# Three chunks of 512 tokens in place of four of 384, units of four query tiles, and the second batch's keys and values loaded late

## The reference

```python
k_sum = k.reshape(B, H, nb, block, D).max(axis=3)
v_sum = v.reshape(B, H, nb, block, D).mean(axis=3)
scores_l = scale * np.matmul(q, k.transpose(0, 1, 3, 2))        # only |i - j| < 16
scores_s = scale * np.einsum('bhsd,bhnd->bhsn', q, k_sum) + np.log(block)
a = softmax(concat(scores_l, scores_s)); x = a @ concat(v, v_sum)

h = np.maximum(x @ w_in, 0.0);  x = h * h @ w_out               # width 2048 inside
h = x @ w_in                                                     # second MLP, width 1024
solu = h * softmax(h)
ln = (solu - mean(solu)) / np.sqrt(var(solu) + 1e-06) * g_ln
out = ln @ w_out
```

## Time and profile before

| | |
|---|---|
| median of three runs | 483.61 us |
| profiled execution | 483.07 us |
| its span, first to last instruction | 481.3 us |
| TensorE busy | 474.0 us, 98% |
| VectorE / ScalarE / GpSimd busy | 253.7 / 207.4 / 30.9 us |
| bytes by DMA | 39.73 MB |
| first up(2) (end of the head) | 33.6 us |
| last `down` ahead of the second MLP ends | 331.6 us |

### The profile page before, as it was taken

How to read it: one execution, slowest core, us unless ns; L and a number is a source line. 1 busy time by engine, 2 the same in 40 slices (tenths; PEclk the granted TensorE clock), 3 DMA queues, 4 the chain that set the end, 5 groups by cost and what they waited for, 6 DMA issues and landing times.

```text
span 481.3 us, 7844 instructions
## 1 busy us (share of the span) xinstructions
PE 474.0 (98%) x2990; PEld 436.1 (91%) x2990; DVE 253.7 (53%) x517; ACT 207.4 (43%) x525; POOL 30.9 (6%) x60
## 2 busy tenths in 40 slices
PE   7999999999999999999999999999999999999997
PEld 5799999899999999999999999999888888888885
DVE  5888787985443444634443424456574444444450
ACT  3986666544343343533433423334353333333341
POOL 2321000240000000000000000000000000000000
PEclk9999999999999999999999999999999999999999
DMA  8999532223211110411000412121122000000001
GB/s 304 290 351 354 153 97 80 87 73 127 70 31 31 57 30 29 161 33 55 1 1 1 133 44 89 44 89 44 56 76 67 24 31 30 26 23 22 23 22 45
DMA packets 27494, 39.73 MB, mean 83 GB/s; under 512 B 2592, under 2 KB 16832, under 8 KB 27456
## 3 DMA queue, kind: packets, MB, share of 16 engines
q1 hardware_dynamic: 27456, 39.22, 25.2%
HBM read 32.77 MB, written 6.29 MB: 81 GB/s over the span
## 4 chain that ended last, share of the span: by engine, by line
PE 86%; issue 7%; DVE 2%; DMA 2%; SPq 1%; ACT 1%; POOL 0%; POOLq 0%; ACTq 0%; DVEq 0%
PE bank L903 25%; PE bank L931 25%; PE bank L1053 13%; PE bank L1026 12%; PE bank L825 4%; PE bank L880 3%; PE bank L1041 2%; PE bank L850 2%; DMA win_raw<-w_in_t 2%; PE bank L859 1%; DVE solu L783 1%; DVE stat L775 1%; DVE lnT_lo L796 0%; SPq L250 0%; PE bank L831 0%
## 5 line engine op out<-in xcount | busy, mean ns | idle before, releaser
L903 PE MATMUL bank<-x_hi,win_hi 128*128 128x384 f32 x256 | 87.7, 343 | 0.0
L931 PE MATMUL bank<-h_hi,wout_hi 128*128 128x384 f32 x256 | 85.9, 335 | 0.0
L903 PE MATMUL bank<-x_hi,win_lo 128*128 128x384 f32 x256 | 85.7, 335 | 0.0
L931 PE MATMUL bank<-h_hi,wout_lo 128*128 128x384 f32 x256 | 85.6, 334 | 0.0
L903 PE MATMUL bank<-x_lo,win_hi 128*128 128x384 f32 x256 | 85.6, 334 | 0.0
L931 PE MATMUL bank<-h_lo,wout_hi 128*128 128x384 f32 x256 | 85.5, 334 | 0.0
L650 DVE TENSOR_TENSOR sqr<-relu 128x384 f32<-128x384 f32 x64 | 35.7, 558 | 88.2 <-ACT relu L490 87.9
L490 ACT ACTIVATE relu<-bank 128x384 f32<-128x384 f32 x64 | 31.5, 492 | 108.5 <-PE bank L903 108.3
L903 PEld LDWEIGHTS bank<-x_hi,win_hi 128*128 128x128 f32 x256 | 48.1, 188 | 0.5 <-DMA q_sb<-qT 0.3
L903 PEld LDWEIGHTS bank<-x_lo,win_hi 128*128 128x128 f32 x256 | 48.1, 188 | 0.0
L931 PEld LDWEIGHTS bank<-h_lo,wout_hi 128*128 128x128 f32 x256 | 48.1, 188 | 0.0
(11 more groups left out here) (78 smaller groups left out, 705.2 us busy)
## 6 DMA issues: line engine op xcount, KB each, us to landing
q_sb<-qT SPq DMA_DIRECT2D x24, 192.0 KB, 2.8
win_raw<-w_in_t SPq DMA_DIRECT2D x8, 512.0 KB, 11.8
wout_raw<-w_out_t SPq DMA_DIRECT2D x8, 512.0 KB, 12.7
win_raw<-w_t SPq DMA_DIRECT2D x8, 512.0 KB, 3.3
v_ext<-vwin SPq DMA_DIRECT2D x24, 144.0 KB, 2.9
k_raw<-kT SPq DMA_DIRECT2D x8, 400.0 KB, 4.2
out<-o_sb SPq DMA_DIRECT2D x12, 256.0 KB, 2.0
v_first<-vrows SPq DMA_DIRECT2D x4, 384.0 KB, 8.3
```

The costliest lines, as they stand in the source:

```text
L903: last = nc.tensor.matmul(up_bank(n), win[a][:, f * WC + k * P:f * WC + (k + 1) * P], x[b][:, c % 2, k * CH:(k + 1) * CH], start=(k == 0 a ...
L931: last = nc.tensor.matmul(down_bank(d), wout[a][:, f * WC + d * P:f * WC + (d + 1) * P], h[b][:, n % 3, :], start=(f == 0 and a == 0 and b ...
```

## The change

CH becomes 512 and TPU 4, so there are 3 chunks, 48 steps and 24 units, still eight to a chunk. VP becomes 4: the second batch's values come in four parts of twice the size. To make room, the first batch's `k_raw` and `v_first` move under `win_hi`; the second batch's keys (`k_next`, for the summaries only), `v_next` and `v_sum` move under `wout_hi` from tile 7 on; `probs` has two buffers, `q_sb` two, `e_sb` one; `lnT_lo` moves. The windows of the second batch's keys are no longer copied by GpSimd but loaded from memory into `k_ext` (`load_kw`). In PSUM all of `up` from step 2 on uses bank 7, and later units' xT has bank 6 for itself. The copies of weights wait for those who used the space before. The orders written out by hand are redone on all engines, and most weight loads move into SyncE's loop over units. The diff, cut to its core (the buffers' declarations and renamed indices are left out):

```diff
-CH = 384
+CH = 512
...
-TPU = 3
+TPU = 4
...
-VP = 8
+VP = 4
...
-V_AT = {4: 0, 6: 1, 7: 2, 8: 3, 9: 4, 10: 5, 11: 6, 12: 7}
-
-VN_BEHIND = {UPC + 2: (1,), UPC + 3: (2, 3), UPC + 4: (4, 5), UPC + 5: (6,), UPC + 6: (7,)}
+K_AT = {1: 0, 3: 1, 5: 2, 6: 3}
+V_AT = {2: 0, 3: 1, 4: 2, 5: 3}
+KTILES = 7
...
         def up_bank(n):
-            return bank[:, 6 + n % 2, 0:CH]
+            return bank[:, 6 if n == 1 else 7, 0:CH]
...
             def load_q(u):
-                sp.dma_start(q_sb[:, u % PPB, :], qT[u, :, :]).then_inc(q_in[u % PPB], 16)
+                if u >= UPC + 2:
+                    sp.wait_ge(scores_ok, u - 1)
+                sp.dma_start(q_sb[:, u % 2, :], qT[u, :, :]).then_inc(q_in[u % 2], 16)
+
+            def load_kn(p):
+                sp.dma_start(k_next[:, p, :], kT[PPB + p, :, MARGIN:MARGIN + S]).then_inc(kn_in[p], 16)
+
+            def load_kw(u):
+
+                row, p = u // PPB, u % PPB
+                sp.wait_ge(scores_ok, u - PPB + 1)
+                dst = k_ext[:, p, :].rearrange("p (t c) -> p t c", t=TPU)[:, :, NB:KX]
+                at = (row % RB) * UQ
+                flat = kT[PPB + p, :, at:at + UQ].rearrange("p (t c) -> p t c", t=TPU)
+                rows, tiles, _ = [list(x) for x in flat.ap]
+                src = bass.AP(flat.tensor, flat.offset, [rows, tiles, [1, WIN]])
+                sp.dma_start(dst, src).then_inc(kw_in[p], 16)
...
+            load_q(UPC + 2)
+            load_kw(UPB)
+            load_vn(0)
+            sp.wait_ge(attn_ps, UPC)
+            sp.wait_ge(vkept_ok, 1)
+            load_kn(0)
+            load_kn(1)
+            load_q(UPC + 3)
+            load_kw(UPB + 1)
+            load_w(win_raw, w_in_t, 3, win_in)
+            load_w(wout_raw, w_out_t, 2, wout_in)
+            load_kn(2)
+            load_kn(3)
             for u in range(UPC, UNITS):
                 if u >= 2 * UPC and u % UPC == 0:
                     save_y(u // UPC - 2)
                 sp.wait_ge(attn_ps, u + 1)
                 if u + PPB < UNITS:
+                    load_vw(u + PPB)
                     load_q(u + PPB)
-                    load_vw(u + PPB)
-                if UPB - PPB - 3 <= u < UPB - 3:
-                    p = u - (UPB - PPB - 3)
-                    sp.wait_ge(kwin_ok, UPB - PPB + p + 1)
-                    load_k(1, p)
-                for j in VN_BEHIND.get(u, ()):
-                    load_vn(j)
+                if UPB <= u + PPB + 2 < UNITS:
+                    load_kw(u + PPB + 2)
+                if u == UPC:
+                    sp.dma_start(g_sb[:, :], g_cols).then_inc(g_in, 16)
+                    load_vn(1)
+                for g in range(4 + 2 * (u - UPC), min(6 + 2 * (u - UPC), F1 // WG)):
+                    load_w(win_raw, w_in_t, g, win_in)
+                    load_w(wout_raw, w_out_t, g - 1, wout_in)
+                if u == UPC + 1:
+                    load_vn(2)
+                    load_w(wout_raw, w_out_t, F1 // WG - 1, wout_in)
+                if u == UPC + 2:
+                    load_vn(3)
                 if u == UPB - 1:
...
-                        windows_k(u)
+                        if u < UPB:
+                            windows_k(u)
...
-                if u >= UPC:
-
-                    act.wait_ge(masked_ok, min(u + 3, UNITS))
-                    act.wait_ge(probsT_ps, min(u + 2, UNITS))
...
             def w_in_high(f):
+
+                if f == 3:
+                    act.wait_ge(vmean_ps, PPB)
+                if f == 9:
+                    act.wait_ge(kwin_ok, UPB)
                 act.wait_ge(win_in[f // WG], 16)
                 nc.scalar.copy(win_hi[:, tile_cols(f)], win_raw[:, tile_cols(f)]).then_inc(win_hi_ok, 1)
 
             def w_out_high(f):
                 if f == 1:
                     act.wait_ge(attn_ps, UPC)
+
+                if KTILES <= f < KTILES + 6:
+                    act.wait_ge(ksum_ok, PPB + ((f - KTILES + 1) * WC - 1) // S + 1)
+                if f == KTILES + 6:
+                    act.wait_ge(vavg_ok, 1)
+                if f == F1 - 1:
+                    for p in range(PPB):
+                        act.wait_ge(vs_in[p], 16)
...
             exps(0)
             exps(1)
             copy_mean(0)
+            copy_mean(1)
+            copy_probsT(0)
+            w_in_high(0)
+            w_in_high(1)
             exps(2)
-            copy_probsT(0)
-            copy_mean(1)
-            w_in_high(0)
...
             def sums_k(b, p):
-                dve.wait_ge(k_in[p], 16 * (b + 1))
                 if b:
                     dve.wait_ge(kbc_ok, p + 1)
-                nc.vector.tensor_reduce(k_sum[:, p, :],
-                                        k_raw[:, p, MARGIN:MARGIN + S].rearrange("p (n b) -> p n b", b=BLOCK),
-                                        AX.X, ALU.max).then_inc(ksum_ok, 1)
+                    dve.wait_ge(kn_in[p], 16)
+                else:
+                    dve.wait_ge(k_in[p], 16)
+                src = k_next[:, p, :] if b else k_raw[:, p, MARGIN:MARGIN + S]
+                nc.vector.tensor_reduce(k_sum[:, p, :], src.rearrange("p (n b) -> p n b", b=BLOCK), AX.X, ALU.max)\
+                  .then_inc(ksum_ok, 1)
...
             def maxima(u):
                 row = u // PPB % RB
-                s, kind = u % 3, 0 if row == 0 else 2 if row == RB - 1 else 1
+                s, kind = u % 2, 0 if row == 0 else 2 if row == RB - 1 else 1
                 if u == 0:
                     dve.wait_ge(mask_in, 16)
                 if u == 2 * PPB:
                     dve.wait_ge(edge_in, 16)
                 dve.wait_ge(scores_ok, u + 1)
-                if u >= 3:
-                    dve.wait_ge(probsT_ps, u - 2)
+                if u >= 2:
+                    dve.wait_ge(probsT_ps, u - 1)
...
+                if n in K_AT:
+                    sums_k(1, K_AT[n])
                 if n in V_AT:
                     sums_v(V_AT[n])
...
                 if 2 <= u <= UPC:
                     pe.wait_ge(masked_ok, u - 1)
-
-                pe.wait_ge(kwin_ok, u + 1)
+                elif u > UPC:
+                    pe.wait_ge(masked_ok, u)
+                if u < UPB:
+                    pe.wait_ge(kwin_ok, u + 1)
+                else:
+                    pe.wait_ge(kw_in[p], 16 * (row - RB + 1))
...
-                        pe.wait_ge(relu_ok, n - 1)
+                        pe.wait_ge(relu_ok, 1 if n == 2 else n)
                 for k in parts:
```

More of the change, by code:

```diff
@@ L90, in build @@
         x_lo = sb(ctx, "x_lo", [P, 2, XC], F32R)
+        first = ExitStack()
+        sb(first, "first_tiles", [P, 3 * WC], F32)
+        v_first = sb(first, "v_first", [P, PPB, SK * P], F32)
+        k_raw = sb(first, "k_raw", [P, PPB, SE], F32)
+        first.close()
         win_hi = sb(ctx, "win_hi", [P, F1 * WC], F32R)
@@ L96, in build @@
         raw.close()
+        late = ExitStack()
+        sb(late, "late_tiles", [P, F1 * WC], F32R)
+        lnT_lo = sb(late, "lnT_lo", [P, 2, FF2], F32R)
+        late.close()
         win_lo = sb(ctx, "win_lo", [P, F1 * WC], F32R)
@@ L106, in build @@
         early.close()
+        second = ExitStack()
+        sb(second, "second_tiles", [P, KTILES * WC], F32)
+        k_next = sb(second, "k_next", [P, PPB, S], F32)
+        v_next = sb(second, "v_next", [PPB * NB, VD * BLOCK], F32)
+        v_sum = sb(second, "v_sum", [PPB * NB, P], F32)
+        second.close()
         wout_hi = sb(ctx, "wout_hi", [P, F1 * WC], F32R)
@@ L124, in build @@
         att = ExitStack()
[L126 to L129, removed]
+        q_sb = sb(att, "q_sb", [P, 2, TPU * P], F32)
         k_ext = sb(att, "k_ext", [P, PPB, UC], F32)
@@ L156, in build @@
         mask_in, edge_in, ident_in, g_in = sem("mask_in"), sem("edge_in"), sem("ident_in"), sem("g_in")
-        q_in = [sem(f"q_in{p}") for p in range(PPB)]
+        q_in = [sem(f"q_in{i}") for i in range(2)]
+        kn_in = [sem(f"kn_in{p}") for p in range(PPB)]
+        kw_in = [sem(f"kw_in{p}") for p in range(PPB)]
         k_in = [sem(f"k_in{p}") for p in range(PPB)]
@@ L527, in _ @@
             copy_probsT(6)
-            w_in_high(2)
+            w_out_high(0)
             x_high(6)
@@ L750, in _ @@
                         normalise(SLOTS[h][2])
-                for h in (2 * n - 2, 2 * n - 1):
-                    if h in SLOTS and SLOTS[h][2] is not None and UPB <= SLOTS[h][2] + 2 < UPB + PPB:
-                        sums_k(1, SLOTS[h][2] + 2 - UPB)
+                if n in K_AT:
+                    sums_k(1, K_AT[n])
                 if n in V_AT:
@@ L946, in _ @@
             scores(1)
+            means(0)
+            means(1)
+            turned(0)
             scores(2)
-            means(0)
-            turned(0)
-            means(1)
             scores(3)
             turned(1)
+            means(2)
             scores(4)
@@ L957, in _ @@
             values(1)
-            scores(6)
-            means(2)
             turned(3)
             means(3)
+            scores(6)
```

(6 more changed lines are left out.)

150 lines of the change are left out of this document (70 added, 80 removed).

## The result

The changed kernel takes 487.78 us in the median of five runs (487.21 to 489.44) beside 483.95 us for the kernel before. The ratio is 1.0087, with the 95% interval 1.0068 to 1.0106: 0.9% slower, where no change was forecast, and outside the forecast's own range of 481.5 to 486 us. Its profiled execution took 488.26 us, with a span of 486.5: 5.2 us more than the span of before.

A forecast was written before the change was run, and what follows sets the result against it. TensorE, busy 98% of the span, was taken as the bound, with all three engines close to full in the head. 483.07 + 5.4 head - 13.8 middle + 1.3 down blocks + 7.1 wait = 483.1; median 483.6, own range 481.5 to 486.

The forecast's parts named there:

- TensorE loses 7.1 us: Middle, at values(12): the second batch's spread values come at 54.0 us after T0, due at 46.9; about 1.1 already at up(8).
- The queue: Middle: 5.64 MB of loads up to vn(2) take 15.9 us at 354 GB/s plus 2.0; there 41.1 us after T0.
- T0: Start of up(2), where the head ends; 33.59 us before the change, forecast 39.0, +5.4, bounds +3.8 and +8.5.
- Slots: Attention work between up and down in the middle: 1.70 us each before, forecast 2.21, bounds 1.70 and 2.27.
- The head's waits: Head, from ScalarE's weight copies at 14.75 to x_high(7) at 35.4: 19.5 us of work plus 1.1 of waits.
- a T0 after 41: Sign, at the end of the head, that the rival of the head scaling as a whole holds; forecast 39.0.
- Wider matmuls: First MLP: 384 fewer matmuls at 13.3 ns fixed cost, 5.1 us saved; a block of 12 takes 2.72 us.
- the last stage: Behind the middle: two down blocks go from 4.18 to 5.44 us, +1.3; the second MLP otherwise unchanged.
- Keys from memory: Second batch's keys: twelve loads replace twelve GpSimd copies, costing nothing, or at most 1 us in a backlog.
- Values in time: Rival, middle: the second batch's values avoid the backlog, only 0.7 of 7.1 us stays; 477.2 us, chance 0.20.
- The head as a whole: Rival, head: the probability ring sets the pace, eight units cost 3.1 us more, +8.5; 486.7 us, chance 0.28.
- the ring of two: Head: with two probability buffers maxima(u) waits for turned(u-2), 2.3 us a unit against 2.5 of ScalarE work; mechanism of a rival, 0.28.

The follow-up runs named there:

- e3_fill: Changed kernel plus unread matmuls while TensorE waits: 9 ahead of up(8), 27 ahead of values(12); 487.31 us, ratio 1.0071 to the kernel before.
- e6_fill2: Changed kernel plus unread matmuls while TensorE waits, with 20 instead of 27 ahead of values(12); 485.53 us, ratio 1.0042 to the kernel before.
- e9_earlier: Changed kernel with weights from w_in 3 and w_out 2 issued behind load_vn(0), before SyncE's first wait, and GpSimd's v_ext copy held back; 482.69 us, ratio 0.9985.
- e1_swap: Changed kernel with vn(2) issued ahead of unit 9's four weight loads instead of behind them; 485.5 us, ratio 1.0042 to the kernel before.
- e4_latecopy: Changed kernel with GpSimd's copy of the first batch's values to v_ext held back until maxima(8); 486.77 us, ratio 1.0056 to the kernel before.
- e2_early: Changed kernel with the nine weight groups of SyncE's unit loop issued at once behind load_kn(3); 478.22 us, ratio 0.9889 to the kernel before.
- e7_probs3: On top of e2_early, a third buffer of probabilities for the first eight units; 478.27 us, ratio 0.9876 to the kernel before.
- e5_best: Changed kernel with the edits of e2_early and e4_latecopy, and value sums one step earlier; 477.61 us, ratio 0.9876 to the kernel before.

## Why the forecast was wrong

The text before named the mechanism of the loss (vn(2) behind eight weight loads, VectorE standing still, the spread values late) and the runs confirm it. The two stops were shared out otherwise than it said: 3.1 us at up(8) and 3.3 at values(12), for 1.1 and 6.0. What failed were three terms.

*A term was missing: the clock behind a stop of TensorE.* The step "TensorE loses 7.1 us" ended when the values came. In the run profiled the slot and `up` behind it took 3.0 us more (7.9 for 4.9). `e3_fill` and `e6_fill2` show that it is the stop that costs this. It came again behind the stop of 5.4 us in `e9_earlier` (1.7 us) and that of 3.9 us in `e1_swap` (slot and `up` 6.4 us for 4.9). What the other four executions paid is not shown: their mean clock was 0.993, not 0.988, and `e4_latecopy`, at 0.993 as well, paid nothing. In the median the gain of `e6_fill2` says 2.2.

*The queue was too fast in the sum.* vsum(1) was done at T0 + 23.3 (forecast 23.1), but the part was there at T0 + 43.2 and not 41.1: 19.9 us for the 5.64 MB instead of 18.0. The 351 and 354 GB/s of the earlier trace rows were the rates of a backlog already standing. The windows of the kernel after show 192 GB/s from 64 to 68 us, where SyncE still issues the loads, 339 and 358 in the next two, 387 only from 76 to 80, and 280 from 80 to 84. That is some 6.2 MB, more than the 5.64 up to vn(2): loads issued behind it were already moving beside it. Which of the two counts for more, the slow start or this sharing, stays open. values(12) came at T0 + 55.6 (forecast 54.0), a stop of 8.7 us by the prediction's own due time of T0 + 46.9, for 7.1. Slots and small waits being 1.4 us cheaper than forecast in sum (what is left over here; `e2_early` shows the same, with a middle of 283.6 us for the 284.9 that the prediction gives it with its values in time), the middle misses by 1.6 + 3.0 - 1.4 = 3.2.

*The head's waits were too small.* The prediction had T0 at 39.0; it was 41.13. ScalarE's weight copies start at 14.99 (forecast 14.75), so 0.2 of it is the loads. From there to the end of x_high(7), at 37.5 instead of 35.4, the forecast had 19.5 us of work and 1.1 of waits, and the waits came to 3.0 if the work was as forecast. 0.84 of these are the GpSimd copy beside normalise(5), as `e4_latecopy` shows. Some 1.1 us is left open: neither a third buffer nor an earlier key load moved it. The prediction named a T0 after 41 as the sign of its rival on the head. T0 was 41.13, and `e7_probs3` shows that the sign misled.

What held:
- *Wider matmuls.* 2.72 us a block in the whole middle. So 13.3 ns of each matmul is there at 512 columns too, beside relu and square. By the fixed cost of 2.5 ns in the Trainium skill, TensorE: Matmul & The Clock Gate ("Wait — 56ns, not 53.3ns?"), a block would be, as an estimate, 12 x (213.3 + 2.5) = 2.59 us; no such block is here.
- *Slots* 2.13 for 2.21, *the last stage* +1.2 for +1.3.
- *Keys from memory.* No wait for `k_ext` of the second batch stands in the waits.
- *Values in time*, the rival at 477.2 us: made true by `e2_early`, with 478.22 in the median. The rival's profiled execution would be 476.7, and it took 477.1: the head was 1.9 longer than forecast and the middle 1.3 shorter, so a part of the nearness is luck.
- *The head as a whole*, at 486.7: the size of the head fell between it and the forecast (+7.5 for +5.4 and +8.5), its mechanism, the ring of two, was refuted by `e7_probs3`. That the median came within 1.1 us of the rival's time is luck.

## What to carry to other kernels

Loads that wait for a buffer should not stand behind bulk loads in one in-order queue; put the bulk ahead of the first such wait, but behind the small loads that are due soonest (`e2_early` won 9.6 us on the kernel after; `e9_earlier`, with the weights ahead of one wait and six small loads more, is 4.5 us slower than that, and level with the kernel before). When a forecast has TensorE stop, add what the lower clock costs behind the stop: here 1.7 us behind one of 5.4 us, 3.0 us behind the two of 3.1 and 3.3, and nothing where the slow work fell ahead of a wait that was due anyway. For a backlog that is yet to build up, take the rate of its start as well as the rate of a full queue.

## What the runs showed of the hardware

At the lower clock a matmul of 512 columns is paid by its columns alone. Starts on TensorE's timeline behind the first stop, 1.2 GHz granted:

```profile
86.80 0.63 PE L960 MATMUL bank<-x_lo,win_hi 128*128 128x512 f32 x1
87.23 0.63 PE L960 MATMUL bank<-x_hi,win_lo 128*128 128x512 f32 x1
87.66 0.63 PE L960 MATMUL bank<-x_hi,win_hi 128*128 128x512 f32 x1
88.08 0.63 PE L960 MATMUL bank<-x_lo,win_hi 128*128 128x512 f32 x1
```

1.28 us for three is 427 ns each, and 512 columns at 1.2 GHz are 426.7 ns. At 2.4 GHz it is 226.7, which is 13.3 more than the columns. The fixed part shows only at the upper clock. The same section of TensorE: Matmul & The Clock Gate, in the Trainium skill, states just this (start to start is the columns at 1.2 GHz, with a fixed cost at the upper clock alone); the rows agree with that and not with its size. Whether the 13.3 ns lie in the weight loads was not tried.

A GpSimd copy of 24 x 2048 numbers held up a VectorE multiplication of 128 x 480: 1.44 us instead of 0.65. By the two rows above, the copy runs from 26.23 to 28.12 and the multiplication ends at 28.63, half a microsecond behind the copy's end, which looks like being stopped rather than slowed. The maximum at 26.62, which reads one tensor from SBUF, ran beside the same copy and took its usual 0.65 us. SBUF — State Buffer in the Trainium skill ("SBUF: two separate sides") has a rule for this: a VectorE operation with two inputs in SBUF and a GpSimd operation that reads SBUF exclude each other for a whole instruction. The trace agrees roughly: the one instruction with two such inputs was held up, and 0.65 us from the copy's end would be 28.77.

A stop of TensorE of 1.6 us (`e5_best`) left the mean clock at 1.000, and behind the one of 2.2 us in `e4_latecopy` it was 1.00 as well. The stops of 3.1 and 3.3 us (kernel after), 3.3 (`e4_latecopy`, at up(8)), 3.9 (`e1_swap`, mean clock 0.996) and 5.4 us (`e9_earlier`) were each followed by the lower level.
